# Nine steps of a triangular solve put together ahead of one mask in a Trainium2 recurrence kernel

## What is computed

```python
for t in range(S):
    y[:, :, t] = np.einsum('bhd,bhde->bhe', rt, state)
    Sa = np.einsum('bhde,bhe->bhd', state, at)
    state_decay = state * wt[:, :, None, :] - np.einsum('bhd,bhe->bhde', Sa, bt)
    state = state_decay + np.einsum('bhd,bhe->bhde', vt, kt)
```

## Time and profile before

| what | value |
|---|---|
| median of 3 runs | 925.05 us (922.23 to 927.7) |
| profiled execution, its own time | 923.58 us |
| its span from first to last instruction | 921.9 us |
| PE busy | 824.6 us, 89% of the span |
| PE weight loads busy | 597.0 us, 65% |
| DVE busy | 559.7 us, 61% |
| ACT busy | 317.4 us, 34% |
| POOL busy | 259.5 us, 28% |
| mean granted clock of TensorE | 0.946 |

### The profile page before, as it was taken

How to read it: one execution, slowest core, us unless ns; L and a number is a source line. 1 busy time by engine, 2 the same in 40 slices (tenths; PEclk the granted TensorE clock), 3 DMA queues, 4 the chain that set the end, 5 groups by cost and what they waited for, 6 DMA issues and landing times.

```text
span 921.9 us, 27713 instructions
## 1 busy us (share of the span) xinstructions
PE 824.6 (89%) x11872; PEld 597.0 (65%) x11872; DVE 559.7 (61%) x1235; ACT 317.4 (34%) x741; POOL 259.5 (28%) x525
## 2 busy tenths in 40 slices
PE   3428989998999988889998999988999998999988
PEld 3428889988998988864465654545644656545555
DVE  8995795878599742136528645357464277354474
ACT  4102331323133232222227542246432266322364
POOL 2087777778778877000000000000000000000000
PEclk9999895979599798899999999999999979999999
DMA  3645575657566574620100000100001000000000
GB/s 117 153 85 122 126 163 113 134 139 140 122 157 138 113 158 102 157 78 26 44 1 15 16 15 1 43 0 23 15 8 43 1 8 22 16 1 0 1 15 30
DMA packets 130922, 61.33 MB, mean 67 GB/s; under 512 B 106544, under 2 KB 119792, under 8 KB 130800
## 3 DMA queue, kind: packets, MB, share of 16 engines
q1 hardware_dynamic: 96156, 32.61, 16.3%
q10 hardware_dynamic: 34644, 26.95, 11.3%
HBM read 45.37 MB, written 14.16 MB: 65 GB/s over the span
## 4 chain that ended last, share of the span: by engine, by line
PE 75%; DVE 11%; issue 5%; ACT 5%; POOL 2%; DMA 1%; SPq 0%; ACTq 0%; DVEq 0%
PE ps_all L808 8%; PE ps_all L792 8%; PE ps_scan L105 5%; PE ps_all L852 5%; PE ps_scan L188 4%; PE ps_all L918 4%; PE ps_all L900 4%; PE ps_all L930 4%; PE ps_scan L130 3%; PE ps_scan L167 3%; PE ps_all L795 3%; PE ps_all L802 2%; PE ps_all L835 2%; PE ps_scan L122 2%; PE ps_scan L114 2%
## 5 line engine op out<-in xcount | busy, mean ns | idle before, releaser
L328 POOL TENSOR_TENSOR t_update<-solver_then_w_down 128x133 f32<-128x133 f32 (+13 forms) x251 | 118.6, 473 | 88.1 <-DMA solver_then_w_down<-l_blocks 39.1
L330 POOL TENSOR_TENSOR solver_then_w_down<-solver_then_w_down,t_update 128x133 f32<-128x133 f32 (+13 forms) x251 | 132.7, 529 | 19.7
L105 PE MATMUL ps_scan<-decayed_a_and_eye,scaled_then_x 40*128 40x104 f32 x768 | 67.6, 345 | 46.5 <-DVE decayed_a_and_eye L362 45.2
L1129 DVE TENSOR_REDUCE minus_max<-ps_all 128x1 f32<-128x128 f32 (+5 forms) x96 | 55.3, 617 | 66.8 <-PE ps_all L904 66.8
L105 PEld LDWEIGHTS ps_scan<-decayed_a_and_eye,scaled_then_x 40*128 40x128 f32 x768 | 62.8, 252 | 48.6 <-issue 47.7
L808 PE MATMUL ps_all<-gated,solver_then_w_down 128*128 128x384 f32 x256 | 91.1, 499 | 0.0
L792 PE MATMUL ps_all<-scaled_then_x,inputs_then_w_up 128*128 128x384 f32 x256 | 88.8, 490 | 1.8 <-ACT ak_l_then_ffn L970 1.8
L1028 ACT ACTIVATE probs_t<-ps_all 128x512 f32<-128x512 f32 (+3 forms) x128 | 55.1, 452 | 69.9 <-PE ps_all L918 69.3
L808 PEld LDWEIGHTS ps_all<-gated,solver_then_w_down 128*128 128x128 f32 x256 | 46.0, 189 | 44.6 <-issue 19.1
L792 PEld LDWEIGHTS ps_all<-scaled_then_x,inputs_then_w_up 128*128 128x128 f32 x256 | 47.6, 190 | 36.3 <-ACT ak_l_then_ffn L970 6.0
L232 ACT ACTIVATE x_rhs<-ps_scan 128x320 f32<-128x320 f32 x48 | 21.0, 438 | 141.3 <-PE ps_scan L122 70.5
(11 more groups left out here) (117 smaller groups left out, 1523.8 us busy)
## 6 DMA issues: line engine op xcount, KB each, us to landing
r_t_and_v_t<-in_rv ACTq DMA_DIRECT2D x48, 160.0 KB
inputs_then_w_up<-in_x ACTq DMA_DIRECT2D x46, 160.0 KB
solver_then_w_down<-l_blocks SPq DMA_DIRECT2D x22, 256.0 KB, 4.6
uv_and_ruv<-in_v ACTq DMA_DIRECT2D x48, 80.0 KB, 3.7
y_t<-y_out SPq DMA_DIRECT2D x24, 160.0 KB
out<-out_rows SPq DMA_DIRECT2D x24, 160.0 KB, 1.8
inputs_then_w_up<-in_x ACTq DMA_DIRECT2D x46, 81.4 KB
inputs_then_w_up<-in_x ACTq DMA_DIRECT2D x46, 80.0 KB
```

What stands on the lines that cost most here:

```text
L105: last = nc.tensor.matmul(PS[:, o:o + ROWS], weights, AL[c % NK][rows(h), p, :], start=True, stop=True)
L328: return (lambda: eng.tensor_tensor(tmp[:, 0:cols, 0:rest], l[:, s:s + 1, s + 1:BLK].broadcast_to(shape), t[:, 0:cols, s:s + 1].broadcast_ ...
L330: lambda: eng.tensor_tensor(t[:, 0:cols, s + 1:BLK], t[:, 0:cols, s + 1:BLK], tmp[:, 0:cols, 0:rest], ALU.subtract))
L1129: nc.vector.tensor_reduce(NM[:, v:v + 1], PS[:, first_bank(v) * 512:first_bank(v) * 512 + n], AX.X, ALU.min).then_inc(m["nm"], 1)
```

## The change

`solve_head` loses its arguments and always issues nine steps; `hm(n - 1)` follows them. Turn 1 was so already. The constant `FIRST` goes, so the lines of the functions shown are numbered one lower in the changed kernel, and those behind the loop of `vector` four lower.

```diff
-FIRST = 4
...
-        def solve_head(j, steps, last):
-            if steps.start == 0:
-                dve.wait_ge(m["l_in"], 32 * j)
-                dve.wait_ge(m["eye"], j + 1)
-                if j == 2:
-                    dve.wait_ge(m["solved_first"], 1)
-                else:
-                    dve.wait_ge(m["head"], j - 2)
-            for s in steps:
+        def solve_head(j):
+            dve.wait_ge(m["l_in"], 32 * j)
+            dve.wait_ge(m["eye"], j + 1)
+            if j == 2:
+                dve.wait_ge(m["solved_first"], 1)
+            else:
+                dve.wait_ge(m["head"], j - 2)
+            for s in range(HEAD):
                 mult, sub = step(nc.vector, LU[j % 2], TS[j % 2], TMD, s)
                 link(dve, mult())
-                if s < last:
+                if s < HEAD - 1:
                     link(dve, sub())
                 else:
                     sub().then_inc(m["head"], 1)
...
             if n % 2 == 1 and 2 <= pair < NPAIR:
-                first = HEAD if pair == 2 else FIRST
-                solve_head(pair, range(0, first), HEAD - 1)
+                solve_head(pair)
                 hm(n - 1)
-                solve_head(pair, range(first, HEAD), HEAD - 1)
                 if ahead: gm(g)
```

## The result

| | before | changed |
|---|---|---|
| median of 10 runs each, same chip | 923.64 us (917.34 to 943.87) | 929.27 us (920.55 to 933.7) |
| profiled execution, own time | 923.58 us | 927.68 us |
| its span | 921.9 us | 926.0 us |
| mean granted clock in it | 0.946 | 0.948 |

The ratio of the changed kernel to the one before is 1.0121, 95% interval 1.0083 to 1.0159. The medians of all runs differ by 0.61% and the means by 4.4 +- 5.3 us, which alone would not tell the two kernels apart.

A forecast was written before the change was run, and what follows sets the result against it. PE bounds the kernel, with three quarters of the span, so other engines matter where they stop it. Mask stalls 7.2, T waits -2.0 and one clock fall 4.6 gave +9.8 us on the 925.05 median, rounded 935.0 us, range 926 to 944.

The forecast's parts named there:

- Which way and how much: Whole kernel: +9.8 us, 1.1% slower; forecast case chance 0.42, slower in all 0.68.
- The mask where h is ready: PE's L105 in turns 7, 9, 13, 15 and 17 waits for the later mask: 7.2 us of new idle time.
- The mask where h is late: Turns 3, 5 and 11: five steps, 2.8 us, fit into DVE's idle time for h; cost nothing.
- From DVE's end to PE's start: Delay between DVE ending the mask and PE going on: 0.06 us taken for each of five waits.
- Turn 19: L188 waits for the mask there; taken as no cost, with a 1.7 us stall kept for the range.
- POOL and T: Earlier heads start POOL sooner; PE's waits for T in turns 19 and 20 close, -2.0 us; POOL idle 9 to 13.
- Steps beside POOL: DVE steps slowed by POOL: at most 1.3 us in one turn, only turns 9 and 11; taken as nothing.
- The clock: New PE stalls bring one more fall to clock 0.50 in turns 7 to 18: +4.6 us.
- my own sign: The prediction is wrong if the number of clock falls in the changed trace is the same or smaller.
- Absorbed: Rival: PE's issue gaps before L122 in even turns vanish, 1.84 us come back, 928.4 us; chance 0.15.
- Faster: Rival: T comes back sooner, its waits and one clock fall go, mask not late for L105: 918.4 us; chance 0.09.

The follow-up runs named there:

- late-turn kernel: Kernel before, with nine steps ahead of the mask of h in turns 13 to 19 alone: +3.8 +- 3.7 us, ratio 1.0043.
- the kernel with nine ahead in the early turns: Kernel before, with nine steps ahead of the mask of h in turns 3 to 11 alone: +4.2 +- 3.5 us, ratio 1.0021.
- the pair with both loads moved: Kernel before and changed kernel, each with up weights moved to turn 20 and down weights to turn 23: ratios to before 0.9981 and 1.0069.
- the change again: The changed kernel as it is, rerun against the kernel before in the second group: +6.1 +- 2.5 us, ratio 1.0109.

## Why the prediction was right, and where not

**Which way and how much: right.** Slower by 9.9 us was the sum's 7.2 - 2.0 + 4.6, rounded. The ratio says 11, the means of all runs 4 to 6 us. The first two terms hold; the third was too large, and a term was missing. These two errors are of opposite sign and of like size (some 3.6 us too much for the clock, 3.9 us of waiting for V left out), so that the total fits as well as it does is luck; that PE waits for the late mask, and that this makes most of the loss, is not.

**The mask where h is ready: right in size, less so in place.** Forecast 7.2 us in turns 7, 9, 13, 15 and 17. Measured 5.7 us in the first profile, in turns 3, 9, 11, 15 and 17, and 8.0, 8.4 and 7.7 us in three other kernels with the same order on DVE. Turns 7 and 13 did not wait in the first profile and did in others (13 in the late-turn kernel, 1.0 us). Whether a turn waits depends on how far DVE is ahead of PE when it gets there, and that on the clock of the turn before. My turn by turn list was one draw of it. The sum over the turns is the steadier quantity.

**The mask where h is late: wrong for turns 3, 5 and 11.** I costed them at nothing behind a cover of 0.1 to 0.9 us. In turn 11 there was no cover at all: I took the 2.8 us of turn 7's five steps, and those of turn 11 took 2.95 (mask ends 233.93, ninth step ends 236.88) against 2.88 us of idle time. Turn 3 waited 0.64 us and turn 11 1.46 in the first profile, turn 5 2.37 in the kernel with nine ahead in the early turns. Such a thin cover should have been given a price. It was made up for by the turns that did not wait, which is luck too.

**From DVE's end to PE's start: right.** 0.06 us taken, 0.05 seen in turn 9 (197.99 to 198.04).

**Turn 19: right.** There is no wait for the mask of h in turns 18 to 23 of the changed kernel.

**POOL and T: right for T, not for POOL's idle time.** The 2.0 us before L130 in turns 19 and 20 are gone from the changed profile. POOL's idle time fell to 22.1 us, not to the 9 to 13 that I gave. In turns 7 and 9 its wait fell from 3.93 and 3.31 us to 0.20 and 0.52, but in turns 11, 15, 17 and 19 it grew (3.06, 3.34, 1.97 and 3.90 against 1.97, none, 1.40 and 3.62). I had treated the nine waits as independent; a pair that starts sooner also ends sooner, and part of the idle time comes back before the next head. That last step is my reading of the rows and not tested.

**Steps beside POOL: too small a price in one turn, right in the sum.** In turn 9 the nine steps took 6.1 us (190.65 to 196.79) in place of 5.1 before (202.01 to 208.41, less the mask), with POOL at work until 196.35, and the 1.32 us wait there is above the 1.01 that the sum had. Over turns 3 to 17 they took 44.9 us in place of 43.6, so the steps were beside POOL about as much as before. That only turns 9 and 11 have POOL still busy was misread: turn 15 has it too, by the same paragraph's own row. The Trainium skill (SBUF — State Buffer, Who interferes with whom) would have had the loser blocked for a whole instruction each time. The multiply of the first step took 0.37 us there and 0.19 in turn 19 of the kernel before, so what is lost lies under the 0.4 us that this would give.

**The clock: the step that was mis-sized.** I took "one more fall, +4.6 us". At the place it was even an understatement. In all eight kernels that waited for the mask of h at L105 or L104, 26 of these waits were of 1.0 us or more, and in the 8 us behind each the granted clock was 0.79 or less (in one of them it had been 0.77 in the 8 us before, too); of eleven waits of 0.56 to 0.83 us six had such a stretch behind them. But falls behind the waits took the place of others, or were short. In the first pair of profiles the changed kernel was granted 0.87 over the recurrence against 0.86, and the kernel before had two long stretches (138 to 162 and 230 to 252 us, at or near 0.50) that the changed one has not. Counted in steps of 1 us below 0.75, the kernel before has 9 stretches of 89 us in all and the changed one 12 of 85; the pair with both loads moved has 10 of 70 and 9 of 69. So by my own sign (a number of falls that is the same or smaller) the clock's part of the mechanism is not borne out: more stretches in one pair, fewer in the other, no more time at the lower clock in either. Over the runs the clock was 0.0017 lower in the change again, 1.2 us, and 0.001 lower in the change of the pair with both loads moved, both within their error of 0.004. So what the term should have been is about +1 us, give or take 3, a balance and not a count. Why the long stretches of before did not come is not shown.

**V: missing.** I had asked what a head that ends sooner sets free on POOL and left out what POOL sets free on SP: the weights, which stand behind T on that queue. A PE held up by the mask comes to the same collision. 3.9 us of waiting for V in the first profile, 6.3 in the change again. Its share of the time is not settled: taking it away makes the changed kernel faster by 0.4% on one comparison of ratios (1.0109 and 1.0069) and 0.7% on the other (1.0040), across chips, with intervals of 0.3 to 0.4% each.

**Absorbed:** not seen before L122, not excluded elsewhere. PE's own issue gaps there came to 5.4, 6.0 and 8.6 us in three kernels with four ahead and to 6.7, 4.5, 6.6 and 7.7 us before L121 in four with the change. All issue gaps from 80 to 410 us came to 18.3, 16.5 and 20.1 us against 15.7, 10.9, 16.6 and 19.3: some 2.7 us less on average, with a spread as large. **Faster:** T did come back sooner and did remove its two waits; the mask was late for L104, so the case did not arise.

What stays open: V's exact share, whether part of the new waits is absorbed in PE's issue gaps, and the size of the loss within 0.5 to 1.2%. The clock makes one run differ from the next by more than the effect.

## What to carry to other kernels

When a piece of work that another engine waits for is moved behind work that nobody waits for yet, the two ends simply change places: read where the last of the group ends now, subtract where the other engine wants it, and do it for every turn, with thin covers priced too. An order on a nearly full engine has a cost on either side. Here putting four of nine steps ahead of the mask used the idle time before h without passing it, and none, two or nine were all slower. And when something upstream ends sooner, follow it to the last queue: a large load that stood behind it may now go ahead of, or right behind, a small one that the busiest engine needs.

## What the runs showed of the hardware

Matmuls with 40 rows that alternate between the lower and the upper half of the array's rows took 2.04 us for 32 records at a granted clock of 1.00 and 3.74 us at the lower clock; the same matmuls issued one half after the other took 3.46 us (turn 12) and 6.42 us (turns 8 and 16). Only their order and the place of the wait for the mask were changed. The Trainium skill (TensorEngine Tiling (Array Packing), Key Properties) says that different tiles of the array can load weights and multiply in parallel. The traces agree: the 768 records of L104 last 338 ns each on average and keep PE busy for 65.9 us in all in the changed kernel, 344 ns and 115.9 us in the other order. The kernel with that order was 4% slower than the changed kernel by the ratios (1.0525 / 1.0109, on two chips).

A small load (V) issued 1.0 to 2.5 us after 1.3 to 1.5 MB of weights, on another queue, was used 6.8 to 9.0 us after its issue in the seven cases in which PE waited for it; issued 0.9 to 1.7 us ahead of the weights, 5.8 to 8.2 us after (five cases); issued 5.1 us ahead of them, 4.9 us after (the kernel before).

And each of the 26 waits for the mask of 1.0 us or more, with work close before and behind it, was followed by a stretch at the lower clock, without the change as a whole being granted less clock (0.87 against 0.86 over the recurrence). It is no rule for every wait of that length: of PE's some 90 other waits of 1.0 us or more in these profiles (95 to 402 us) about one in five had a granted clock above 0.85 in the 8 us behind it, such as 1.26 and 1.38 us in the kernel with no step ahead (128.68 and 226.29, clock 1.00 before and behind).
